# Linear attention with a gated mixture of experts: order of the copies on ScalarE, of the state's sum and of the chain steps on VectorE

## The reference

```python
# part 1: gated linear attention with complex decays ar + i ai; B, H, S, D = 4, 8, 768, 48
for t in range(S):
    S_re, S_im = ar * S_re - ai * S_im + k_t v_t, ar * S_im + ai * S_re
    y[:, :, t] = q_t S_re
x = y as 3072 tokens of 384
# part 2: x @ w_in (1024 wide), SoLU, layer norm, @ w_out
h = x @ w_in
solu = h * exp(h - max h) / (sum + 1e-9)
x = (solu - mean) / sqrt(mean((solu - mean) ** 2) + 1e-6) * g_ln @ w_out
# part 3: mixture of 8 experts, each token takes its best two
logits = x @ w_gate + log1p(exp(x @ w_noise)) * noise
out = sum over the two of weight * relu(x @ w1[e]) @ w2[e]
```

## Time and profile before

| | us |
|---|---|
| median of three runs (1211.77 to 1214.28) | 1214.07 |
| the profiled execution | 1212.83 |
| its span, first to last instruction | 1211.1 |
| busy PE, DVE, ACT, POOL | 1041.4, 872.8, 621.1, 449.7 |

### The profile page before, as it was taken

One profiled execution on the slowest core, in us unless ns is written; L12 is line 12 of the kernel. 1 busy time (PEld: TensorE's weight loads), 2 busy tenths in 40 slices (PEclk: granted clock), 3 DMA queues, 4 the chain that ended last, 5 costly groups with the idle time before them and its releaser, 6 DMA issues.

```text
span 1211.1 us, 21883 instructions
## 1 busy us (share of the span) xinstructions
PE 1041.4 (86%) x7866; PEld 984.5 (81%) x7866; DVE 872.8 (72%) x1729; ACT 621.1 (51%) x967; POOL 449.7 (37%) x417
## 2 busy tenths in 40 slices
PE   0046988988998998899964999999999999999996
PEld 0035887877887887788864999999999999999996
DVE  6888779879969969945553777667676767776672
ACT  6432663764664664544532555555555555555551
POOL 4110241252352352243523244345434533543442
PEclk9977998998898898899986999999999999999998
DMA  9420220230230210211404666767676767676640
GB/s 231 174 76 27 54 86 27 67 86 27 66 87 27 64 37 27 58 42 53 125 14 156 227 233 226 253 234 256 202 267 235 253 227 244 228 230 235 209 162 1
DMA packets 85980, 167.51 MB, mean 138 GB/s; under 512 B 18566, under 2 KB 57696, under 8 KB 85872
## 3 DMA queue, kind: packets, MB, share of 16 engines
q1 hardware_dynamic: 72432, 137.71, 36.1%
q0 software_dynamic: 13440, 28.40, 6.4%
HBM read 148.83 MB, written 21.92 MB: 141 GB/s over the span
## 4 chain that ended last, share of the span: by engine, by line
PE 55%; issue 2%; ACT 1%; DVE 1%; DMA 1%; POOL 0%; POOLq 0%; DVEq 0%; ACTq 0%; SPq 0%
PE bank L1367 22%; PE bank L1547 21%; PE bank L1411 3%; PE bank L1358 3%; PE bank L1459 3%; PE bank L1433 1%; PE bank L1491 1%; PE bank L1471 0%; ACT z L859 0%; DMA xg<-xs,mine 0%; PE bank L1477 0%; PE bank L1387 0%; DMA tags<-tag,idx 0%; ACT x L856 0%; ACT x2t L867 0%
## 5 line engine op out<-in xcount | busy, mean ns | idle before, releaser
L899 ACT ACTIVATE hh<-bank 128x256 fp32r<-128x256 f32 x248 | 95.3, 384 | 256.6 <-PE bank L1367 256.6
L1367 PE MATMUL bank<-sxh,w1h 128*128 128x256 f32 x744 | 212.1, 285 | 2.1 <-DVE sxl L1317 2.1
L1367 PE MATMUL bank<-sxh,w1l 128*128 128x256 f32 x744 | 210.3, 283 | 0.0
L1367 PE MATMUL bank<-sxl,w1h 128*128 128x256 f32 x744 | 210.0, 282 | 0.0
L1336 DVE SCALAR_TENSOR_TENSOR hl<-bank,hh 128x256 fp32r<-128x256 f32 x248 | 104.8, 423 | 120.8 <-ACT hh L899 109.0
L672 POOL DMA_INDIRECT out<-yo,mine x62 | 77.9, 1256 | 277.8 <-DVE yo L1329 268.4
L1547 PE MATMUL bank<-w2h,hh 128*128 128x384 f32 x496 | 167.4, 337 | 0.0
L1547 PE MATMUL bank<-w2l,hh 128*128 128x384 f32 x496 | 166.8, 336 | 0.0
L1547 PE MATMUL bank<-w2h,hl 128*128 128x384 f32 x496 | 166.6, 336 | 0.0
L1367 PEld LDWEIGHTS bank<-sxh,w1h 128*128 128x128 f32 x744 | 140.8, 189 | 2.5 <-DVE sxl L1317 2.5
L1367 PEld LDWEIGHTS bank<-sxh,w1l 128*128 128x128 f32 x744 | 141.5, 190 | 0.0
(11 more groups left out here) (184 smaller groups left out, 2353.4 us busy)
## 6 DMA issues: line engine op xcount, KB each, us to landing
raw<-in_w SPq DMA_DIRECT2D x62, 1536.0 KB
ar<-in_a_re SPq DMA_DIRECT2D x6, 768.0 KB, 4.7
turn<-in_a_im SPq DMA_DIRECT2D x6, 768.0 KB, 7.0
qk<-in_q SPq DMA_DIRECT2D x48, 96.0 KB, 2.4
qk<-in_k SPq DMA_DIRECT2D x48, 96.0 KB, 2.5
out<-wide SPq DMA_DIRECT2D x9, 512.0 KB, 11.3
vt<-in_v SPq DMA_DIRECT2D x24, 192.0 KB, 2.6
xs<-x SPq DMA_DIRECT2D x24, 192.0 KB, 2.7
```

The source lines that it names most:

```text
L899: nc.scalar.activation(hh[:, f % NH, :], bank[:, f % 2, 0:CAP], ACT.Relu).then_inc(hh_done, 1)
L1367: ins = MM(dst, stationary[a_](cc), moving[b_](cc), start=(n_ == 0), stop=(n_ == len(terms) - 1))
```

## The change

It makes five edits. On ScalarE the copy of the turned result, and in b = 3 the first inverse ahead of it, go ahead of centring, and Square goes behind high x. Square writes into a buffer of its own in SBUF, `squared`, and no more over the banks of the hidden product. On VectorE the sum into the state goes right behind the softmax product and the mean, ahead of what was `fill(6)` and, in b = 3, of the f2 sums. That `fill` is gone; ahead of low x at most ten steps are made there, and the rest of the share behind the q products. On TensorE the hidden product waits for the mean of the tile before (`solu_step`) instead of for its variance.

```diff
--- before.py
+++ after.py
@@ -158,6 +158,7 @@
         mv = [m1(f"mv{i}", [P, 3]) for i in range(2)]
         rstd = [m1(f"rstd{i}", [P, 2]) for i in range(2)]
         mhalf = m1("mhalf", [P, 2])
+        squared = m1("squared", [P, F])
         g_sb = m1("g_sb", [P, FC])
         wg = m1("wg", [P, KC, 2 * E])
         nz = m1("nz", [P, T, E])
@@ -854,25 +855,24 @@
                     if j >= 2:
                         act.wait_ge(x_sent[par], 16 * (j // 2))
                     nc.scalar.activation(x2[par][:], bank[:, 0, 0:DM], ACT.Copy, scale=rstd[par][:, 1:2]).then_inc(x2_evac, 1)
-                if has(i):
-                    act.wait_ge(solu_step, 4 * i + 4)
-                    nc.scalar.activation(z[:], z[:], ACT.Identity, bias=mv[i % 2][:, 1:2]).then_inc(centred, 1)
-
-                    act.wait_ge(centred, i + 1)
-                    nc.scalar.activation(bank[:, 4:6, :].rearrange("p b x -> p (b x)"), z[:], ACT.Square,
-                                         accum_out=mv[i % 2][:, 2:3]).then_inc(var_done, 1)
+                if b == 3 and prep:
+                    inverse(2 * c + 2)
                 if has(j):
                     act.wait_ge(x2t_mm, j + 1)
                     wait(act, lg_mm, j)
                     nc.scalar.activation(x2t[:].rearrange("p c t -> p (c t)"), bank[:, 3, 0:DM], ACT.Copy).then_inc(x2t_evac, 1)
-                if b == 3 and prep:
-                    inverse(2 * c + 2)
+                if has(i):
+                    act.wait_ge(solu_step, 4 * i + 4)
+                    nc.scalar.activation(z[:], z[:], ACT.Identity, bias=mv[i % 2][:, 1:2]).then_inc(centred, 1)
                 if has(m):
                     act.wait_ge(y_mm, m + 1)
                     if m == 0:
                         act.wait_ge(w_ready, 2)
                     wait(act, h_mm, m)
                     nc.scalar.activation(xh[0:PR].rearrange("p c t -> p (c t)"), bank[0:PR, 7, :], ACT.Copy).then_inc(xt_hi, 1)
+                if has(i):
+                    act.wait_ge(centred, i + 1)
+                    nc.scalar.activation(squared[:], z[:], ACT.Square, accum_out=mv[i % 2][:, 2:3]).then_inc(var_done, 1)
                 if ahead:
                     scale(2 * c + 2)
                     scale(2 * c + 3)
@@ -1247,20 +1247,19 @@
                     fill()
                     dve.wait_ge(solu_step, s0 + 3)
                     V.tensor_scalar(mv[par][:, 1:2], mv[par][:, 0:1], -1.0 / F, None, ALU.mult).then_inc(solu_step, 1)
-                fill(6)
-                if b == 3 and prep:
-                    f2(2 * c + 2)
-                    f2(2 * c + 3)
                 if 0 <= m < LIVE:
 
                     apart(dve, (w_mm, m + 1), (state_step, 3 * (m - B + 1)), (wide_done, 2 * (m - B + 1)))
                     V.tensor_tensor(state[:, m % B].rearrange("p s n e -> p (s n e)"),
                                     state[:, m % B].rearrange("p s n e -> p (s n e)"),
                                     bank[:, 6, 0:2 * NP * D], ALU.add).then_inc(w_added, 1)
+                if b == 3 and prep:
+                    f2(2 * c + 2)
+                    f2(2 * c + 3)
                 if has(n):
                     weigh(n)
                     k_products(n)
-                fill(share - made[0])
+                fill(10)
                 if has(m):
                     dve.wait_ge(xt_hi, m + 1)
                     wait(dve, h_mm, m)
@@ -1268,6 +1267,7 @@
                                     xh[0:PR].rearrange("p c t -> p (c t)").bitcast(F32), ALU.subtract).then_inc(xt_lo, 1)
                 if has(n):
                     q_products(n)
+                fill(share - made[0])
                 if n == 0:
                     weights_scaled()
                     weights_rest(0)
@@ -1417,7 +1417,7 @@
                 if has(i):
                     pe.wait_ge(w_ready, 2)
                     pe.wait_ge(xt_lo, i + 1)
-                    wait(pe, var_done, i)
+                    wait(pe, solu_step, 4 * i)
                     hidden(0, 6 * NP)
                 if has(m):
```

## The result

The changed kernel takes 1206.03 us (median of nine runs, 1203.07 to 1208.95) where the kernel before takes 1211.73 us beside it (nine runs, 1208.63 to 1214.28). The ratio is 0.9952, with a 95% interval of 0.9936 to 0.9969: 5.7 us less, and faster by more than the 0.2% of the prediction. The forecast was 4.1 us less. It named 1210.0 us, counted from a median of 1214.07; 2.3 of the 4.0 us between 1210.0 and 1206.03 are that the kernel before, too, was faster in the nine runs.

The account below looks back on a forecast made before the run. VectorE's queue was taken to bound the middle chunks, TensorE the last chunk and tail. First chunk -2.4, four chunks +0.8, four tiles -0.4, tail -2.1 sum to -4.1 us: 1210.0 us, range 1205.5 to 1219.0.

Parts of the forecast that it names:

- What bounds: Middle chunks: one queue of VectorE work from quarter 1's low z through quarter 3; TensorE alone bounds last chunk and tail.
- First chunk, -2.4: Tile 1's low x 2.4 us early, won at VectorE's wait for tile 2's hidden product; bounds -0.5 and -4.0.
- Quarter 0, +0.6: First body of each chunk: later Square delays GpSimd's power and the low z behind it, +0.6 us; bounds 0 and +1.1.
- rival 3: ScalarE's delays are hidden, quarters 0 and 3 cost nothing; -8.5 us in sum, 1205.6 us; chance 0.12.
- Square's 0.12 us: Square writing SBUF instead of PSUM takes 1.15 us for 1.03, +0.12 each; on the path only in quarter 0.
- Quarter 1, 0: Second body: TensorE's 3.96 us wait goes, low x 1.35 us early, but VectorE reaches the next low z unchanged.
- Quarter 2, -0.9: Third body: earlier hidden product lets the exponential start early, shrinking VectorE's 1.32 us wait; -0.9 us, bounds -1.1 and +0.6.
- rival 2: Cold hidden product in quarter 2 only, 1.7 us a chunk; sum +1.9 us, 1216.0 us, no change; chance 0.22.
- Quarter 3, +0.5: Last body of a chunk: inverse waits for a later f2, delaying ScalarE's copy and centring; +0.5 us, bounds 0 and 1.6.
- Tail, -2.1: Behind the last tile: turning z starts earlier, then the gate behind Square ends at 619.7 against 621.80; -2.1 us.
- Rival 1: Clock takes it back: cold hidden products in quarters 2 and 3, 2.7 us a chunk; +5.9 us, 1220.0 us; chance 0.18.
- Rival 4: Change does little: waits removed in quarters 1 and 3 are replaced, first chunk gives nothing, only tail's -2.1; 1212.0 us; chance 0.08.

Follow-up runs that it names:

- warm8: Changed kernel plus eight extra matmuls ahead of the hidden product in quarters 2 and 3 from the second chunk on; 1202.58 us, ratio 0.9950.
- square_psum: Changed kernel with Square writing PSUM banks 4 and 5 again and the hidden product waiting for Square; 1202.77 us, ratio 0.9948.
- s_only: Kernel before with only ScalarE's new order, Square's own buffer and TensorE's wait for the mean; VectorE's order unchanged; 1206.65 us, ratio 0.9932.
- v_only: Kernel before with VectorE's edits alone; ScalarE and TensorE keep their order; 1204.77 us, ratio 0.9942.
- v_tail: Kernel before with VectorE's edits, plus the copy of the turned result ahead of centring behind the last tile only; 1203.17 us, ratio 0.9948.
- f2_first: Changed kernel with the two f2 sums of quarter 3 ahead of the state's sum again; 1199.40 us, ratio 0.9909.
- tail_only: Kernel before with the copy of the turned result ahead of centring behind the last tile alone; 1210.14 us, ratio 0.9965.
- first_chunk: Kernel before with at most ten steps ahead of low x, the rest behind the q products, in the first chunk alone; 1209.48 us, ratio 0.9964.
- best: Changed kernel with quarter 0's old centring and Square order, f2 sums ahead of the state, last Square behind its zh copy; 1197.41 us, ratio 0.9900.

## Why the prediction came out as it did

The sign and the size by the medians (5.7 for 4.1 us) were right, and so were what bounds and the two places where the gain sits, the first chunk and the tail, both too small. Part of the rest is luck: in the sum of a chunk, quarter 0 (+0.6) and quarter 2 (-0.9) were both wrong, with opposite signs, and cancelled. By low z the places sum to 4.6 and 2.5 us, and the medians give 5.7; the difference is within the interval of the ratio.

**What bounds.** Right. Bringing TensorE's work forward by 2 us in warm8 gave the middle chunks nothing. The low-z wait of quarter 1 grew from 4.0 to 4.2 us, and 0.8 us stand at high x in quarter 3, both as written. But the bound isn't tight: with ScalarE's edits alone a chunk is 1.2 us shorter, in quarters 2 and 3.

**First chunk, -2.4.** The mechanism is right and the size too small. Low x of tile 1 is 2.4 us early as worked out, and of the three carry steps of tile 2, which I kept as a bound of -4.0, another 1.6 to 1.9 us come. The changed kernel is 4.6 us ahead at tile 5, in spite of a loss on the way (next point).

**Quarter 0, +0.6.** In the middle chunks 0.0: from the scaled copy of the result to low z it takes 10.25 us before (339.90 to 350.15) and 10.26 us after (335.01 to 345.27). The step that failed is that Square's end starts GpSimd's power. It does, but GpSimd gets through only when VectorE's q products are over, as the prediction half suspected (the lower bound, 0, and rival 3). Before, they made the power 2.02 us long; in the changed kernel they do the same to the instruction ahead of it:

```profile
339.54 1.45 POOL L636 TENSOR_SCALAR rstd<-mv 128x1 f32<-128x1 f32 x1 [0.78 <-ACT squared L875]
339.66 1.28 DVE L1072 TENSOR_TENSOR qp<-cum,qk 128x512 f32<-128x512 f32 x2
...
341.07 0.57 POOL L639 TENSOR_TENSOR rstd<-rstd,mhalf 128x1 f32<-128x1 f32 x1
341.62 1.83 POOL L559 TENSOR_TENSOR cum<-cum 128x768 f32<-128x768 f32 x1
```

In the chunk from tile 4 it costs 1.9 us, more than the bound of 1.1: the way is 9.10 us before and 10.96 after. There the power had been through ahead of the q products, and the sum of logs ran beside them:

```profile
159.88 0.55 POOL L638 TENSOR_TENSOR rstd<-rstd,mhalf 128x1 f32<-128x1 f32 x1
160.40 3.25 POOL L558 TENSOR_TENSOR cum<-cum 128x768 f32<-128x768 f32 x1
160.66 1.28 DVE L1072 TENSOR_TENSOR qp<-cum,qk 128x512 f32<-128x512 f32 x2
```

Now all of GpSimd's work stands behind them. Every execution with the old order of quarter 0 takes 8.3 to 9.1 us there (eight kernels), every one with the new order 11.0 to 11.3 (six). I had taken one chunk as the pattern of four.

**Square's 0.12 us.** Wrong, it is 0.025. Centring takes its 1.14 us whether Square goes to PSUM or not. It differs from Square also in its function (Identity), in its bias, which is read from `mv`, and in writing over its own input; which of these costs the 0.09 us, no run parts. The Trainium skill (ScalarE: Activation LUTs, Step-by-step: what each stage is for) calls PSUM the faster target for ScalarE. The trace agrees in the sign, by these 0.025 us, and with square_psum at 0.9948 and the changed kernel at 0.9952 the difference is worth nothing here.

**Quarter 1, 0.** Right for VectorE (22.2 us from tile 13 to 14, for 22.1). But "nearly none" for TensorE's wait was wrong: 1.85 us stayed. I had followed the copy of the turned result and overlooked that the logits also wait for the state's sum, which s_only shows as 3.87 us. That it is the state's sum is read from the code and from the times: the logits start at 363.14, the sum in s_only ends at 363.03. So the part of the change that I took for no gain there, the state ahead of six steps, is what lets ScalarE's edit take effect on this wait.

**Quarter 2, -0.9.** Measured -0.1 (23.1 us for 23.2 from tile 14 to 15). My reason assumed that VectorE's wait of 1.32 us was time to be had. Two things stood against it. The product started behind a gap of 2.99 us and ran 7.2 us instead of 6.25, so of the 1.35 us by which it should be early only 0.25 are left at its end (4.9 us behind low z for 5.15); that was rival 2's mechanism, at half its price. And warm8 shows that with the product at full clock nothing is won either: the exponential is early, GpSimd's four instructions are early too, and VectorE's chain steps beside them are slower by as much as the wait was long. The step that failed is "with the product early the exponential is early and VectorE gains it": the same copy of the scores also releases GpSimd. Between the two lies a product that ends at 4.2 to 4.6 us, as in v_only and s_only, with 0.4 to 0.6 us won. What the product of the prediction, at 3.8 us, would have given, no execution shows.

**Quarter 3, +0.5.** Measured +0.3 (26.8 us for 26.5 from tile 15 to 16), followed by 0.3 less up to tile 17. The sum was near and the parts were not. ScalarE's order by itself brings 0.6 us (25.9 us in s_only, for 26.5), VectorE's by itself 0.1 to 0.3 (26.4 and 26.2 in v_tail and v_only); together they lose 1.2 us against f2_first, 0.4 to 1.0 with the quarter behind. This is the term that decides between the changed kernel and a better one.

**Tail, -2.1.** Measured 2.5 in the changed kernel and in tail_only, by the path that was named: softplus and the gate are behind Square, and low z follows the last of them without a wait. The profiled execution has 1 us more there, from a hidden product of tile 25 of 5.7 us instead of 7.3; that is the clock of the one execution. The 0.1 us each of four tiles before it came to 0.1 in all (5.1 us ahead at tile 21, 5.2 at 25).

**Rivals.** Rival 1 (the clock gives back 10 us) didn't come about: the chunk is not longer. Rival 2's slow product in quarter 2 is there, but it only took back what the early start had won. Rival 3 (ScalarE's delays are hidden) holds in quarter 0 of three chunks and not in quarter 3. Rival 4 (the first chunk gives nothing) is ruled out by first_chunk. Of rival 3's sentence on GpSimd, that no row parted contention from other causes, the runs made a finding (last section).

## What to carry to other kernels

An idle stretch of the bounding engine is not yet a gain: ask what else the event that ends it releases, and whether that will then run beside this engine's next instructions and slow them by what the wait cost. Such a gain can have a best place: here half a microsecond earlier helped and two didn't. A repeated pattern has to be read in its first and last instance as well; what is hidden in three chunks can be bare in the fourth. When a change moves several things and gains little, undo them one at a time: here two new orders, each harmless alone, met at one wait and took back most of what ScalarE's had brought in the middle chunks. And before a difference between two traces is explained, compare two executions of the same code in that stretch.

## What the runs showed of the hardware

**VectorE and GpSimd take turns.** A chain step with two operands in SBUF takes 0.36 us alone and 0.89 to 1.20 us beside a GpSimd instruction of 0.94 to 1.09 us, that is, until this one is nearly over. VectorE's `tensor_scalar` on one element a partition is not held: 0.14 us at 374.96, with GpSimd busy beside it. Whether its size or its single operand spares it, no run parts. In the other direction GpSimd's instruction on 128x1 grows from 0.24 to 1.48 us beside a q product. A GpSimd instruction that started 0.12 to 0.30 us ahead of the q products was held by them (339.54 and 155.18 in the changed kernel, 344.50 and 160.40 before, the last taking 3.25 us for 1.8); one that started 0.74 us ahead, v_only's sum of logs at 155.47, took its 1.91 us, and the q products 2.32 for 1.28. The Trainium skill (GPSIMD Engine Reference, 8. Key points) names contention with VectorE instructions of two SBUF inputs, and its page Trainium Architecture — The Big Picture (What this means for kernel authors) calls the shared port an exclusive lock; the traces agree with both, by these numbers.

**The clock of TensorE.** A hidden product takes 5.5 to 5.7 us at a granted clock of 1.00 and 7.2 us at 0.76 behind a gap of 3.0 us filled with next to nothing (0.17 us busy). Executions of the same code differ here: the product of tile 18 takes 6.3 us in the kernel before and 8.1 in tail_only, which differ only behind the last tile, and low z of tile 25 comes at 603.34 and 607.36 us. I read no kernel's worth from one product, and whether the clock is what keeps the parts from adding up fully in best isn't settled.

**Scatter.** The nine runs of the changed kernel span 5.9 us, as much as its whole gain; steps of about 2 us, such as v_tail's, can't be told by a ratio of some four runs to eight or more of the kernel before.
